# The routing work of a pair of tiles, one chunk later in layer 0

## The reference, cut to what matters

```python
def _moe2_ref(x, w_gate, w_output_gate, w1, w2):
    logits = x @ w_gate                                # 14336 x 8
    e_idx = np.argmax(logits, axis=1)
    logits_s = logits - logits.max(-1, keepdims=True)
    probs = np.exp(logits_s)
    probs /= probs.sum(-1, keepdims=True) + 1e-09
    gate_w = probs[np.arange(N), e_idx]
    eom = 1.0 / (1.0 + np.exp(-(x @ w_output_gate)))
    for e in range(E):
        mask = e_idx == e
        h = np.maximum(x[mask] @ w1[e], 0.0)           # 192 -> 1024
        ye = h @ w2[e]                                 # 1024 -> 192
        out[mask] = gate_w[mask, None] * eom[mask, e, None] * ye
...
    x = _moe_ref(x=attn_out.reshape(B * S, D), **moe_kwargs)   # the same without eom
    return _moe2_ref(x=x, **moe2_kwargs)
```

## Time and profile before

| | |
|---|---|
| median of 3 runs | 1402.85 us |
| the profiled execution, its own time | 1415.59 us |
| its span from first to last instruction | 1414.1 us |
| TensorE (PE) busy | 1239.4 us, 88% |
| vector engine (DVE) busy | 861.3 us, 61% |
| ScalarE (ACT) busy | 640.1 us, 45% |
| GpSimd (POOL) busy | 449.5 us, 32% |
| granted TensorE clock, mean | 0.917 |

### The profile page before, as it was taken

How to read it: one execution, slowest core, us unless ns; L and a number is a source line. 1 busy time by engine, 2 the same in 40 slices (tenths; PEclk the granted TensorE clock), 3 DMA queues, 4 the chain that set the end, 5 groups by cost and what they waited for, 6 DMA issues and landing times.

```text
span 1414.1 us, 38068 instructions
## 1 busy us (share of the span) xinstructions
PE 1239.4 (88%) x13162; PEld 1161.7 (82%) x13162; DVE 861.3 (61%) x2298; ACT 640.1 (45%) x1126; POOL 449.5 (32%) x476
## 2 busy tenths in 40 slices
PE   3775773199999999999999982999999999999998
PEld 2765663199999999999999981999999999999997
DVE  3887886359999999977777764333333333333332
ACT  2666664145555555544444441333333333333332
POOL 1366777403333333322222221122222222222222
PEclk9666655599999999999999995999999999999999
DMA  8388665744955585535112314325222233152230
GB/s 231 108 249 264 210 204 165 235 85 125 250 142 148 160 232 143 149 99 149 38 45 45 75 42 118 100 46 147 53 45 45 48 102 95 45 145 51 47 86 24
DMA packets 200663, 169.25 MB, mean 120 GB/s; under 512 B 146911, under 2 KB 179323, under 8 KB 197282
## 3 DMA queue, kind: packets, MB, share of 16 engines
q1 hardware_dynamic: 172320, 102.03, 28.9%
q0 software_dynamic: 26096, 64.50, 14.8%
q10 hardware_dynamic: 2194, 2.06, 0.5%
HBM read 75.69 MB, written 70.80 MB: 104 GB/s over the span
## 4 chain that ended last, share of the span: by engine, by line
PE 76%; DVE 10%; issue 4%; ACT 3%; DMA 2%; POOL 2%; another core or an unknown queue 2%; SPq 1%; POOLq 0%; ACTq 0%; DVEq 0%
PE bank L722 74%; DVE am L945 2%; PE bank L727 2%; POOL rows L468 2%; DVE wslot L1056 1%; DMA wslot<-image 1%; DVE split L1029 1%; DVE wam L1014 1%; ACT conv L566 1%; DVE split L1032 1%; ACT rT L566 1%; ACT rowt L566 1%; DVE rowab L954 0%; SPq L371 0%
## 5 line engine op out<-in xcount | busy, mean ns | idle before, releaser
L722 PE MATMUL bank<-xT,wslot 128*128 128x256 f16 x5040 | 634.8, 273 | 53.6 <-DMA xT<-rows 51.4
L1116 DVE SCALAR_TENSOR_TENSOR hl<-bank,hh 128x512 f16<-128x512 f32 x504 | 348.0, 691 | 402.1 <-ACT hh L655 359.1
L722 PEld LDWEIGHTS bank<-xT,wslot 128*128 128x128 f16 x5040 | 483.5, 98 | 101.6 <-DMA xT<-rows 51.6
L655 ACT ACTIVATE hh<-bank 128x512 f16<-128x512 f32 x504 | 300.6, 596 | 527.8 <-PE bank L722 510.9
L722 PE MATMUL bank<-wslot,hh 128*128 128x192 f16 x4032 | 539.2, 246 | 0.0
L722 PE MATMUL bank<-wslot,hl 128*128 128x192 f16 x2016 | 495.9, 246 | 0.0
L722 PEld LDWEIGHTS bank<-wslot,hh 128*128 128x128 f16 x4032 | 368.9, 98 | 10.6
L554 POOL DMA_INDIRECT out_tokens<-y,idxt x126 | 122.8, 975 | 415.9 <-ACT y L666 348.0
L489 POOL DMA_INDIRECT rows<-rowt,idxp x126 | 132.7, 1053 | 344.6 <-PE bank L722 203.7
L722 PEld LDWEIGHTS bank<-wslot,hl 128*128 128x128 f16 x2016 | 197.2, 98 | 0.0
L468 POOL DMA_INDIRECT rows<-rowab,idxa x96 | 110.1, 1147 | 60.9 <-issue 44.9
(11 more groups left out here) (137 smaller groups left out, 872.8 us busy)
## 6 DMA issues: line engine op xcount, KB each, us to landing
wslot<-image SPq DMA_DIRECT2D x18, 1024.0 KB, 5.5
wslot<-image SPq DMA_DIRECT2D x18, 768.0 KB
image<-split POOLq DMA_DIRECT2D x18, 512.0 KB
image<-split SPq DMA_DIRECT2D x8, 1024.0 KB
image<-split POOLq DMA_DIRECT2D x9, 768.0 KB
xw<-in_x SPq DMA_DIRECT2D x4, 1536.0 KB
stage<-in_moe_w SPq DMA_DIRECT2D x8, 768.0 KB
image<-split SPq DMA_DIRECT2D x8, 768.0 KB
```

Source lines behind the costliest of these rows:

```text
L655: nc.scalar.activation(hh[:, c, :], bank[c][:, :], ACT.Relu).then_inc(hh_out, 1)
L722: return nc.tensor.matmul(o, a, b_, start=start, stop=stop, skip_group_check=True)
L1116: V.scalar_tensor_tensor(hl[:, c, :], bank[c][:, :], 0.0, hh[:, c, :], ALU.max, ALU.subtract).then_inc(hl_out, 1)
```

## The change

On each engine the steps of a pair move one chunk on; they stay in the same tiles, but for the second transposes, which move from the end of tile s=1 to the beginning of the tile s=0 that follows.
- TensorE: `row_T` r=0 from before hidden 3 to behind contract 0 of tile s=1; r=1 behind hidden 0 of the next tile; the logits in front of hidden 2; the ranks behind contract 0.
- ScalarE: the copy of r=1 behind relu 0, the copy of r=0 behind relu 3, the exponential behind the outputs, in front of relu 3.
- Vector engine: the choice and the exponential's arguments behind `hl` 1; the scale of the weights stays behind `hl` 0, so is now ahead of the choice; factor and place together behind `hl` 3, in front of `largest_out`.
- GpSimd: `PACE` from 5, 7, 9 to 6, 8, 10; all three loads of weights are issued ahead of the pair's first scatter; the first image waits for one chunk more.

```diff
-PACE = (5, 7, 9)
+PACE = (6, 8, 10)
...
             with pool.Fori(1, E + 1) as i:
-                next_weights(i, 0)
-                next_weights(i, 1)
+                for piece in range(3):
+                    next_weights(i, piece)
                 scatter_row(i * 2 - 2, 0, 0)
-                next_weights(i, 2)
                 scatter_row(i * 2 - 2, 0, 1)
-                paced(i * (4 * NP) + 6)
+                paced(i * (4 * NP) + 7)
                 next_image(i, 0)
...
+                    relu_hi(t, 0)
                     if placing:
                         row_T(k - 2, 1)
-                    relu_hi(t, 0)
...
                     relu_hi(t, 1)
-                    if placing:
-                        exps(k - 2)
                     if splitting:
                         row_hi(k - 1, 1 - v, i if v else i - 1)
                     relu_hi(t, 2)
                     if late(t, 1):
                         outputs(*before(t, k, s))
+                    if placing:
+                        exps(k - 2)
+                    relu_hi(t, 3)
                     if splitting:
                         row_T(k - 1, 0)
-                    relu_hi(t, 3)
...
                     hidden(t, k, s, x, i, 0)
                     if placing:
-                        row_logits(k - 2)
+                        row_T(k - 2, v, 1)
                     for c in range(1, NP):
                         if late(t, 1):
                             contract(*before(t, k, s), c)
-                        if placing and c == 3:
-                            row_ranks(k - 2)
-                        if splitting and c == 3:
-                            row_T(k - 1, 1 - v, 0)
+                        if placing and c == 2:
+                            row_logits(k - 2)
                         hidden(t, k, s, x, i, c)
                     contract(t, k, s, 0)
+                    if placing:
+                        row_ranks(k - 2)
                     if splitting:
-                        row_T(k - 1, 1 - v, 1)
+                        row_T(k - 1, 1 - v, 0)
...
                     hidden_lo(t, 0)
-                    if placing:
-                        choose_out(k - 2)
-                        exp_in_out(k - 2)
-                        if prep and v == 1:
-                            weights_scale(i + (E - 1), 1, i - 1, 0)
+                    if placing and prep and v == 1:
+                        weights_scale(i + (E - 1), 1, i - 1, 0)
...
                     hidden_lo(t, 1)
                     if placing:
-                        factor_out(k - 2, v)
+                        choose_out(k - 2)
+                        exp_in_out(k - 2)
...
                     hidden_lo(t, 2)
-                    if placing:
-                        place_out(k - 2, v)
                     if prep and s == 1:
                         weights_part(i, v, 0)
                     hidden_lo(t, 3)
+                    if placing:
+                        factor_out(k - 2, v)
+                        place_out(k - 2, v)
                     if measuring:
                         largest_out(k - 1)
```

## The result

| | before | after |
|---|---|---|
| median of 10 runs each, same chip | 1402.18 us (1400.75 to 1404.9) | 1406.14 us (1402.33 to 1410.12) |
| ratio | | 1.0027, 95% interval 1.0014 to 1.004 |
| profiled execution, its own time | 1415.59 us | 1406.18 us |
| its span | 1414.1 us | 1404.6 us |
| from the first to the last hidden of layer 0 | 562.28 us | 563.26 us |

What follows compares the result with a forecast made beforehand. The vector engine's serial list was taken to bound the preparing passes, TensorE the rest of layer 0. Excess 8.6 us less the present 5.9 gave +2.7, carried onto 1402.85 us: 1405.6 us, range 1400.5 to 1409.5 (own case 1403.8 to 1407.5).

Steps and rivals of the forecast that it cites:

- The bound: Layer 0's eight preparing passes: the vector engine's serial list sets the 36.06 us period; behind them TensorE alone bounds.
- The two waits: New vector engine waits: 0.11 us a pass for GpSimd's maximum, 0.25 us a pair for the relu behind the exponential.
- The sum of a pass: Vector engine's preparing pass: work stays 36.06 us, plus 0.11 and 2 x 0.25, gives 36.67 us.
- no change: Rival, chance 0.25: the vector engine's list loses one stall of p per pair, 15 x 0.21 = 3.2 us, giving 1402.4.
- Piece 2 of the staged weights: Load now issued ahead of the pair's first scatter; the 0.8 us wait of wam goes, or is added if late.
- GpSimd and DMA: nothing waits: Scatters one chunk later, index about 2 us later; row buffers are needed again over 20 us on, so no wait.
- Slack: TensorE's first transposes of an undisturbed pair: 0.57 us left before they wait, so 17.75 us a pair stays.
- second transposes: TensorE, one hidden behind the first: copy in time, cost taken as 0; rival that they are late, chance 0.10, 1409.5.
- tail: End of layer 0: factor and place (1.62 us) in front of am and xsl, 2.9 us of cover, cost 0.
- the difference lies outside the loop: Sign of being wrong: the time difference between the kernels is not found in the loop.
- theory Q: From the experiments, not the prediction: p of the kernel before stands still only with the profiler.
- TensorE bound everywhere: Rival, chance 0.10: the list falls below 35.50 us a pass and the whole 5.9 us goes, giving 1397.0.

Runs made afterwards that it cites:

- e4: Changed kernel with the exponential behind relu 3, the scale of the weights behind the choice and GpSimd's part as before: 1400.8 us, ratio to before 0.999.
- e10: Kernel before with the reciprocal of the factor done twice in layer 0, one more dependent step per pair: 1421.29 us, ratio to before 1.0019.
- e1: Changed kernel with GpSimd's part (pacing, third load of weights, first image) as before: 1406.53 us, ratio to before 1.0025.
- e2: Kernel before with GpSimd's part of the change alone: 1403.88 us, ratio to before 1.001.
- e9: Kernel before with the first scatter of each pair held until TensorE's sixth chunk: 1434.45 us, ratio to before 1.0091.
- e11: e4 with the third image store ahead of the pair's last scatter and without its own pacing: 1409.66 us, ratio to before 0.9935.

## Why the prediction was right, and where not

**The bound.** Right. In the preparing passes the vector engine's serial list sets the period: both new waits stand on the chain that ended last, with the waits out of the list the pass falls to TensorE's 35.5 (e4), with a step more it grows (e10), and both move the timed median.

**The two waits.** Right to 0.01 us, 0.11 and 0.25, and e1 against e4 prices them: 15 x 0.25 + 7 x 0.11 = 4.5 us by the list, 5.1 in the profiled layer, 5.7 in the timed medians. Nothing in the diff says "wait"; it came from counting what stood between the exponential's arguments and the `hl` queued behind it.

**The sum of a pass.** This is the step that failed: "the sum of the work stays: 36.06 a pass", hence 36.67. It is 36.08. The list's steps stayed, but one of them got shorter. By the forecast's own signs this is neither right (36.6 to 36.7) nor the sign of being wrong (35.5 to 36.0); it lies just above the latter. Over layer 0 (300 to 850 us) the groups of `p` of the two kernels (xcount | busy, mean ns | idle), first before, then after:

```profile
L910 DVE TENSOR_SCALAR p<-am 128x4 int32<-128x4 int32 x31 | 8.9, 288 | 1.1
```

```profile
L909 DVE TENSOR_SCALAR p<-am 128x4 int32<-128x4 int32 (+1 forms) x31 | 5.3, 172 | 1.1
```

That is 3.6 us less, what the rival "no change" had put at 3.2. It was not an alternative to the forecast's mechanism, both happened. The traces suggest why `p` was freed, and the spacing was to be read beforehand. GpSimd starts the first scatter 1.05 to 1.09 behind the start of `idxp`, in both kernels, and it takes about 1.0. A `p` that starts 0.60 to 0.67 into it takes 0.35 to 0.46, until about the scatter's end; one that starts up to 0.34 into it takes 0.17 to 0.19, in all profiles. Before, these were the rows:

```profile
554.79 0.16 DVE L1006 TENSOR_TENSOR idxp<-pos,bad 128x4 int32<-128x4 f32 x1
...
555.50 0.94 DVE L945 TENSOR_REDUCE am<-y 128x4 f32<-128x768 f32 x1
```

With `hl` 3 between place and `am`, `p` started 1.68 behind `idxp`, 0.62 into the scatter of the earlier trace rows. Now place stands directly in front of `am`, `p` starts 1.10 behind `idxp`, 0.05 into the scatter, and is over in time. It is `tf` that starts 0.60 into it (551.76) and takes 0.39, and the `hl` behind `tf` doesn't need its result, so only 0.10 of that shows (`hl` starts at 551.99, 0.23 behind `tf`; behind the `tf` of 559.58, with no scatter beside it, the next instruction starts after 0.13). The same spacing explains e1 (place in front of `am`, `p` at 0.17 with the old pacing) and e2's pair with 0.36 (`idxp` at 547.21, scatter at 548.26, `p` at 548.89). That it is the order of place and `am` was read from these rows and not tried by itself. The first `p` of the kernel before is another case: at 320.62 it took 0.67, beside the issue of the third load of weights (320.31 to 321.29) and not beside a scatter, and ended with it.

Not every small step stands still at such a place. `tid`, `tf` and `p`, copies and scalings of one input, do in most rows; in the kernel before, a step with two inputs, 0.59 into another scatter, does not:

```profile
549.83 1.03 POOL L489 DMA_INDIRECT rows<-rowt,idxp  x1 [0.54 <-PE bank L722]
...
550.42 0.16 DVE L969 TENSOR_TENSOR mx<-mx,bad 128x4 f32<-128x4 f32 x1
```

The GPSIMD Engine Reference of the Trainium skill, section Key points, says that the two engines share their SBUF interfaces, with contention for steps in a two-port mode or with two SBUF inputs. The stall of `p` agrees with the sharing; the row of `mx` does not show the contention that the page has for two inputs. The page has neither the place nor the length of such a stall.

**Piece 2 of the staged weights.** The 0.8 us wait for `wam` is gone, as said. But two other transfers were late instead: 2.4 us on ScalarE in the second pass, and 1.4 us on TensorE at 501.6, where the weights landed 10.5 us after their issue, beside the staged weights issued from 489.65 on. What happened at the first is in the trace of the changed kernel, on the queues of GpSimd, SyncE and on ScalarE:

```profile
363.13 0.59 POOL L517 DMA_DIRECT2D image<-split  x1
363.39 4.23 SPq L376 DMA_DIRECT2D wslot<-image  x2
370.67 1.58 ACT L587 ACTIVATE split<-stage,winv 128x1536 f16<-128x1536 f32 x1 [2.39 <-DMA image<-split]
...
image<-split POOLq DMA_DIRECT2D x1, 768.0 KB, 7.5
```

The store of the previous image was issued just ahead of two loads for the tiles and took 7.5 us, where it takes 3.6 in six later passes and took 4.5 in the kernel before; ScalarE needed its buffer 2.4 us sooner. GpSimd's new order alone is not the cause: with the order of before the wait is 1.7 us in e1 and 2.4 in e4, and with the new order in the kernel before it is 1.4 (e2). "GpSimd and DMA: nothing waits" was true of the row buffers that the forecast looked at, and not of this one.

**Slack, second transposes, tail.** Right: 0.77 us left (0.57 forecast), no wait at the second transposes, none at the end of layer 0. TensorE's 17.75 stayed.

**The time.** The forecast was 1405.6, the median is 1406.14 on its chip. But the agreement is better than the reasoning behind it, and in part luck. In the profiles layer 0 grew by 1.0 and 0.2 us only (562.28 to 563.26, 562.46 to 562.66), not by 2.7, since `p` gave back much of what the waits took. So most of the measured 3.8 us is not in the profiled layer 0, and "the difference lies outside the loop" was one of the forecast's own signs of being wrong. The timed runs on the first two chips nevertheless behave as if `p` had given nothing back. The column "rest" shows it: kernels without the stall have 842.9 to 845.0, e2 with half of it 842.7, the kernel before 839.9 and 841.8; the kernel before is some 2 to 3 us faster in timed runs than its own profile suggests. That is what theory Q asks for (15 x 0.21 = 3.2). It is weak evidence: each rest rests on one profile, and the kernels without the stall differ by 2.1 among themselves. On the third chip it doesn't hold: e10, with the stall, has 855.0 beside 852.1 to 854.4, and there the change costs nothing measurable. So this stays open: whether the kernel before has its `p` stalls in unprofiled executions, and why the change costs 3.8 us in the first measurement and nothing measurable on the third chip. An edit that takes `p` out of the scatter's way and brings no wait of its own would have to be found for it; e9 was not that.

**A better version.** e11 keeps the changed order but for three things: the exponential and the scale of the weights are moved so that neither wait arises, GpSimd's pace is that of before, and the third image store is earlier. It is 9.2 us faster than the kernel before (0.0065 x 1419), and 8.8 below the changed kernel on the same chip. On the first chip e4, which lacks only the earlier image, gained 1.8; the two were not timed side by side, and their profiled layers differ by 0.3, so how much of the 9.2 is the image's and how much the chip's stays open. So the distance of a chunk was worth something: the forecast's rival "TensorE bound everywhere" needed 0.56 us a pass, and in e4 and e11 the pass got it. Layer 0 of e4 is 5.8 to 6.0 us shorter in the profile than that of the kernel before, where the rival had 5.9; timed it is 1.8, the same gap between profiled and timed as above.

## What to carry to other kernels

When a step is moved down an in-order engine that is nearly full, list for each round trip over another engine what of the own work stands between question and answer; here 0.25 us a pair and 0.11 a pass used up what a chunk of distance had won, and one instruction moved on ScalarE gave most of it back. Check also which small step will stand beside a neighbour's DMA issue, by its distance from the event that starts both: a stall that moves from a step in a dependent chain to one that nobody waits for is a gain that no diff shows. And when the times of transfers or of those who wait for them move, follow the oldest buffer that waits for a store, not only the one whose load moved.

## What the runs showed of the hardware

- The scaling step `p`, 128x4 values from one input, took 0.17 us, and 0.35 to 0.46 if it started 0.60 to 0.67 us into GpSimd's indirect DMA instruction (1.0 us); it ended about with that instruction. Started 0.01 to 0.34 us into it, it took 0.17 to 0.19. A step with two inputs, `mx`, took 0.16 us though it started 0.59 us into it.
- The same image store of 768 KB took 3.6 us in six passes and 7.5 us beside two weight loads, where it held up ScalarE for 2.4 us.
- The same kernel had medians of 1402.6, 1404.25 and 1419.5 us on three chips. The ratio of two kernels was 1.0027 (1.0014 to 1.004) in the first measurement and 0.9997 (0.9977 to 1.0017) on the third chip; the intervals just meet.
